# Attention's loads in step order, the first w1 in four quarters, one early split of A11, and idle products at the start

## The reference

```python
for t in range(S):                      # decaying linear attention
    state = gamma * state + outer(k[t], v[t])
    y[t] = scale * q[t] @ state
x = y as (1536, 512)
P = sinkhorn(exp(x @ w_gate - max))     # 8 rounds, 8 experts
x = sum_e P[:, e] * (relu(x @ w1[e]) @ w2[e])       # w1 512x1024, w2 1024x512
p = domain_probs / rows' sums                        # 4 experts
out = sum_e p[:, e] * (relu(x @ w1[e]) @ w2[e])
```

## Time and profile before

| | |
|---|---|
| median of 3 runs | 1560.71 us (1558.86 to 1561.56) |
| the profiled execution: its time | 1563.57 us |
| its span | 1561.8 us |
| PE busy | 1548.5 us, 99% of the span |
| DVE, ACT, POOL busy | 56%, 29%, 3% |
| attention (to the first product of the experts) | 55.5 us |

### The profile page before, as it was taken

How to read it: one execution, slowest core, us unless ns; L and a number is a source line. 1 busy time by engine, 2 the same in 40 slices (tenths; PEclk the granted TensorE clock), 3 DMA queues, 4 the chain that set the end, 5 groups by cost and what they waited for, 6 DMA issues and landing times.

```text
span 1561.8 us, 21255 instructions
## 1 busy us (share of the span) xinstructions
PE 1548.5 (99%) x8228; PEld 1405.0 (90%) x8228; DVE 881.9 (56%) x1434; ACT 445.8 (29%) x860; POOL 53.3 (3%) x45
## 2 busy tenths in 40 slices
PE   8999999999999999999999999999999999999999
PEld 7888998899889988998999899988998899889988
DVE  5846756546545555464555554667555546455553
ACT  4421322223213222232133122333322223213321
POOL 4400000000000000000000000012000000000000
PEclk9999999999999999999999999999999999999999
DMA  9201001011010010010110100101001011011011
GB/s 318 98 0 55 27 28 55 3 52 55 1 54 30 23 54 26 27 54 0 54 54 0 54 27 28 55 0 55 29 26 55 19 36 54 0 54 54 1 43 66
DMA packets 34699, 67.28 MB, mean 43 GB/s; under 512 B 2256, under 2 KB 2384, under 8 KB 34640
## 3 DMA queue, kind: packets, MB, share of 16 engines
q1 hardware_dynamic: 34064, 66.16, 12.2%
q10 hardware_dynamic: 576, 0.30, 0.1%
HBM read 63.31 MB, written 3.15 MB: 43 GB/s over the span
## 4 chain that ended last, share of the span: by engine, by line
PE 97%; DMA 1%; DVE 1%; ACT 0%; SPq 0%; issue 0%; POOL 0%; DVEq 0%; POOLq 0%
PE bank L1066 17%; PE bank L1065 17%; PE bank L1064 17%; PE bank L1043 15%; PE bank L1047 15%; PE bank L1045 15%; DMA qt_in<-in_q_t 1%; PE bank L926 1%; PE bank L964 1%; DMA k_in<-in_k 0%; PE bank L946 0%; PE bank L1011 0%; PE bank L958 0%; DVE w_lo L625 0%; PE bank L992 0%; PE bank L994 0%
## 5 line engine op out<-in xcount | busy, mean ns | idle before, releaser
L1043 PE MATMUL bank<-x_hi,w_hi 128*128 128x384 f32 x1344 | 450.5, 335 | 4.2 <-DVE w_lo L625 2.3
L1047 PE MATMUL bank<-x_hi,w_lo 128*128 128x384 f32 x1344 | 450.2, 335 | 0.0
L1045 PE MATMUL bank<-x_lo,w_hi 128*128 128x384 f32 x1344 | 450.0, 335 | 0.0
L1066 PE MATMUL bank<-w_hi,h_lo 128*128 128x512 f32 x1152 | 449.2, 390 | 0.0
L1065 PE MATMUL bank<-w_lo,h_hi 128*128 128x512 f32 x1152 | 449.0, 390 | 0.0
L1064 PE MATMUL bank<-w_hi,h_hi 128*128 128x512 f32 x1152 | 448.5, 389 | 0.0
L789 DVE SCALAR_TENSOR_TENSOR acc<-bank,gate,acc 128x512 f32<-128x512 f32 x252 | 189.2, 751 | 374.7 <-PE bank L1066 374.7
L490 ACT COPY ups<-bank 128x384 f32<-128x384 f32 x288 | 138.0, 480 | 908.3 <-PE bank L1047 908.3
L742 DVE TENSOR_TENSOR ups<-bank,ups 128x384 f32<-128x384 f32 x288 | 155.3, 554 | 189.5 <-ACT ups L490 167.8
L1043 PEld LDWEIGHTS bank<-x_hi,w_hi 128*128 128x128 f32 x1344 | 252.9, 188 | 6.9 <-issue 2.6
L1066 PEld LDWEIGHTS bank<-w_hi,h_lo 128*128 128x128 f32 x1152 | 216.2, 188 | 45.0
(11 more groups left out here) (83 smaller groups left out, 503.0 us busy)
## 6 DMA issues: line engine op xcount, KB each, us to landing
w_raw<-in_moe_w SPq DMA_DIRECT2D x47, 1024.0 KB, 5.1
kt_in<-in_k_t SPq DMA_DIRECT2D x12, 256.0 KB, 3.7
qt_in<-in_q_t SPq DMA_DIRECT2D x12, 256.0 KB, 5.8
v_in<-in_v SPq DMA_DIRECT2D x12, 256.0 KB, 6.2
k_in<-in_k SPq DMA_DIRECT2D x10, 256.0 KB, 6.7
out<-acc SPq DMA_DIRECT2D x2, 768.0 KB, 3.5
out<-acc SPq DMA_DIRECT2D x6, 256.0 KB, 2.0
w_first<-in_moe_w SPq DMA_DIRECT2D x1, 1024.0 KB, 5.1
```

The source lines that it names most:

```text
L1043: nc.tensor.matmul(o, w1_hi[:, w, kc, fs], x_hi[:, x, kc, at], start=start and kc == 0, stop=False, skip_group_check=True)
L1045: nc.tensor.matmul(o, w1_hi[:, w, kc, fs], x_lo[:, x, kc, at], start=False, stop=False, skip_group_check=True)
L1047: last = nc.tensor.matmul(o, w1_lo[:, w, kc, fs], x_hi[:, x, kc, at], start=False, stop=kc == 1, skip_group_check=True)
L1066: last = nc.tensor.matmul(o, h_lo[:, f, b, rows], w2_hi[:, f, :], start=False, stop=(n == UC - 1))
```

## The change

1. SP loads in step order: kt, qt, k, v of step s together. `rise` moves from ACT's queue to SP's, ahead of step 2's loads.
2. The first w1 comes as four quarters of 256 KB (128 rows each, semaphore `w1_first`), one behind the loads of each of steps 5 to 8.
3. `warm(n)`: three idle products (`WARM_GAP`) behind score(0), three behind score(1).
4. POOL: `first_w1_sum(0)` ahead of raise_q(10), (1) and (2) behind it, (3) behind raise_q(11). The memset of wg_parts is first in its program.
5. A11 is split by itself: ACT `first_w1_high(0)` behind step 9's state copy (ahead of x_high1(4)), DVE `first_w1_low(0)` behind mask_scores(11), and `up` waits for `a11_ready` for its first product, S2, S3 and S1 get shares of their own.
6. The gate weights' split (ACT and DVE) goes to the beginning, gate2's row sums to behind the third half.

```diff
-WARM = 8
+WARM, WARM_GAP = 8, 3
...
             load_qk(0, 0)
+            load_k(0, 0)
             sp.dma_start(mask[:, :, :, :], ...).then_inc(mask_in, 16)
+            load_v(0, 0)
             for s in range(1, STEPS):
                 c, b = s // BATCH, s % BATCH
-                if s == 8:
-                    load_w1(moe_w1, 0, 0)
+                if s == 2:
+                    sp.dma_start(rise[1][:, :, :], ...).then_inc(rise_in, 16)
                 if c > 1:
                     sp.wait_ge(y_done, s - 4 + 1)
                 load_qk(c, b)
-                load_kv((s - 1) // BATCH, (s - 1) % BATCH)
-            load_kv(CH - 1, 1)
+                load_kv(c, b)
+                if 5 <= s < 5 + DC:
+                    at = slice((s - 5) * P, (s - 4) * P)
+                    sp.dma_start(w1_raw[:, s - 5, :], moe_w1[0, at, 0:UF]).then_inc(w1_first, 16)
...
+            for s in range(BATCH, STEPS - BATCH):
+                raise_q(s)
+                decay_k(s)
+            first_w1_sum(0)
+            raise_q(STEPS - 2)
+            first_w1_sum(1)
+            first_w1_sum(2)
+            raise_q(STEPS - 1)
+            first_w1_sum(3)
             sums_low(CH - 1)
...
+            def first_w1_high(part):
+                if part == 0:
+                    act.wait_ge(w1_first, 16 * DC)
+                    nc.scalar.copy(w1_hi[:, W_A11, :, :], w1_raw[:, 0:2, 0:2 * P]).then_inc(a11_hi, 1)
...
+                if s == STEPS - 3:
+                    first_w1_high(0)
...
+                if s == STEPS - 2:
+                    first_w1_low(0)
+                if s == STEPS - 1:
+                    first_w1_low(1)
+                    first_w1_low(2)
...
-            split_w1_low(0, 0)
-            split_w1_low(0, 1)
             x_low0(CH - 1)
...
             score(0)
+            warm(WARM_GAP)
             for s in range(STEPS):
                 if s < STEPS - 1:
                     score(s + 1)
+                if s == 0:
+                    warm(WARM_GAP)
                 attend(s)
...
-                    if p == 0:
+                    if p == 0 and not first:
                         pe.wait_ge(w1_ready, ...)
+                    elif first and n == 0:
+                        pe.wait_ge(a11_ready, 1)
+                    elif first:
+                        pe.wait_ge(w1_ready, {W_S2: 1, W_S3: 1, W_S1: 2, W_S4: 3}.get(w, 4))
```

More of the change, by code:

```diff
@@ L179, in retention_moe_moe_kernel @@
         pool_chain = sem("pool_chain")
+        w1_first = sem("w1_first")
+        a11_hi = sem("a11_hi")
+        a11_ready = sem("a11_ready")
         w1_in = sem("w1_in")
@@ L349, in sums_low, with first_w1_sum @@
                                         ALU.subtract).then_inc(x_lot, 1)
+            def first_w1_sum(n):
+                a11, a21 = w1_raw[:, 0:2, 0:2 * P], w1_raw[:, 0:2, 2 * P:4 * P]
+                a12, a22 = w1_raw[:, 2:4, 0:2 * P], w1_raw[:, 2:4, 2 * P:4 * P]
+                s2, s3, s4 = w1_sum[:, 0, :, :], w1_sum[:, 1, :, :], w1_sum[:, 2, :, :]
+                if n == 0:
+                    pool.wait_ge(w1_first, 16 * DC)
+                else:
+                    pool.wait_ge(w1_summed, n)
+                if n == 0:
+                    nc.gpsimd.tensor_tensor(s3, a11, a21, ALU.subtract).then_inc(w1_summed, 1)
+                elif n == 1:
+                    nc.gpsimd.tensor_tensor(a21, a21, a22, ALU.add).then_inc(w1_summed, 1)
+                elif n == 2:
+                    nc.gpsimd.tensor_tensor(s2, a21, a11, ALU.subtract).then_inc(w1_summed, 1)
+                else:
+                    nc.gpsimd.tensor_tensor(s4, a12, s2, ALU.subtract).then_inc(w1_summed, 1)
+            nc.gpsimd.memset(wg_parts[:, :, :].bitcast(F32), 0.0).then_inc(wg_zeroed, 1)
             pool.wait_ge(kdecay_in, 16)
@@ L452, in split_w1_high, with gate_weights @@
                                    col_halves[:, 2:4, :, :]).then_inc(w1_hi_ready, 1)
+            def gate_weights():
+                act.wait_ge(wg_in, 16)
+                act.wait_ge(wg_zeroed, 1)
+                nc.scalar.copy(wg_parts[:, :, 0:E1], wg_raw[:, :, :]).then_inc(wg_hi_ready, 1)
             act.wait_ge(zeroed, 1)
             nc.scalar.copy(act_warm[:, 1:2], act_warm[:, 0:1])
+            gate_weights()
             for s in range(STEPS):
@@ L458, in _ @@
                 if s == STEPS - 1:
-                    split_w1_high(0, 0, first=True)
+                    first_w1_high(1)
+                    first_w1_high(2)
                 if b == 1:
@@ L493, in hidden_high @@
                 nc.scalar.activation(h_hi[:, f, b, :], src, ACT.Relu).then_inc(h_hi_ready, 1)
[L495 to L498, removed]
             def unit(k, p, x2=None, first=False):
@@ L640, in w1_sums, with first_w1_low @@
                 nc.vector.tensor_tensor(s4, a12, s2, ALU.subtract).then_inc(w1_summed, 1)
+            def first_w1_low(part):
+                if part == 0:
+                    dve.wait_ge(a11_hi, 1)
+                    low(w1_lo[:, W_A11, :, :], w1_raw[:, 0:2, 0:2 * P], w1_hi[:, W_A11, :, :]).then_inc(a11_ready, 1)
+                elif part == 1:
+                    dve.wait_ge(w1_hi_ready, 1)
+                    low(w1_lo[:, W_S2:W_S3 + 1, :, :], w1_sum[:, 0:2, :, :],
+                        w1_hi[:, W_S2:W_S3 + 1, :, :]).then_inc(w1_ready, 1)
+                else:
+                    dve.wait_ge(w1_hi_ready, 2)
+                    low(w1_lo[:, W_S1, :, :], w1_raw[:, 0:2, 2 * P:4 * P], w1_hi[:, W_S1, :, :]).then_inc(w1_ready, 1)
             def split_w1_low(k, part):
@@ L678, in _ @@
             mask_scores(0)
+            dve.wait_ge(wg_hi_ready, 1)
+            low(wg_parts[:, :, E1:2 * E1], wg_raw[:, :, :], wg_parts[:, :, 0:E1]).then_inc(wg_lo_ready, 1)
             for s in range(STEPS):
@@ L698, in _, with gate2_rows @@
             split_w1_low(0, 3)
[L699 to L707, removed]
+            def gate2_rows():
+                dve.wait_ge(gate2_in, 16)
+                then_wait(nc.vector.reduce_sum(row_sum[:, :], gate2[:, :, :], axis=AX.X))
+                then_wait(nc.vector.tensor_scalar_add(row_sum[:, :], row_sum[:, :], EPS))
+                then_wait(nc.vector.reciprocal(row_sum[:, :], row_sum[:, :]))
+                then_wait(nc.vector.tensor_tensor(gate2[:, :, :], gate2[:, :, :],
+                                                  row_sum[:, :].unsqueeze(2).to_broadcast([P, NSUB, E2]), ALU.mult))
             def gate_logits():
@@ L967, in attend, with warm @@
                 last.then_inc(y_done, 1)
+            def warm(n):
+                for i in range(n):
+                    nc.tensor.matmul(bank[7][:, 0:P], state[1][:, 0, :], state[1][:, 0, :], start=True, stop=True)
             pe.wait_ge(zeroed, 4)
-            for i in range(WARM):
-                nc.tensor.matmul(bank[7][:, 0:P], state[0][:, 0, :], state[0][:, 0, :], start=True, stop=True)
+            warm(WARM)
             score(0)
+            warm(WARM_GAP)
             for s in range(STEPS):
```

37 lines of the change are left out of this document (12 added, 25 removed).

## The result

The changed kernel took 1556.5 us in the median of 9 runs (1555.95 to 1557.1) against 1560.7 us (1558.86 to 1562.22, 9 runs) for the kernel before: a ratio of 0.9974 with a 95% interval of 0.9964 to 0.9984, 4.2 us less. The forecast was 1554.5 in a range of 1552.6 to 1558.6, so the time lies in the range, faster as forecast, by two thirds of the 6.2 us. On two later occasions, with new runs of both, the difference was 3.1 and 3.3 us (ratio 0.9980, interval 0.9970 to 0.9989, 10 runs of the change; ratio 0.9982, interval 0.9973 to 0.9991, 11 runs).

What follows compares the result with a forecast made beforehand. PE, busy 99% of the span, bounds the kernel: its work, idle stretches and low clock. Terms 0.9 + 1.6 - 0.3 + 2.3 + 1.7 + 0 = 6.2 us, off the median 1560.7, gave 1554.5 us, range 1552.6 to 1558.6.

Steps and rivals of the forecast that it cites:

- A22's product: End of the first up: PE's wait for DVE, 1.0 us before, about stays; 0 us counted.
- From the median, 1560.7 - 6.2: Last step: the 6.2 us summed from the profiled execution's ledger, taken off the median, giving 1554.5 us.
- start of attention: First scores: idle products and a later qt cost, filled gaps and a full clock give back; 0.9 us gained.
- waits for loads in mid-attention: At score(8): with w1 in quarters qt lands in time and PE's wait goes; 1.6 us gained.
- end of attention: ACT's A11 copy and POOL's third sum delay the last mask, so attention ends 0.3 us later.
- wait for w1's low part: Before the first up: A11's low part is ready before attention's last product, so PE's wait goes; 2.3 us gained.
- clock behind it: Behind attention, 55 to 60 us: without the idle 2.3 us PE's clock doesn't fall; 1.7 us gained.
- rival B: Steps 5 to 9 stay bound by loads at 278 GB/s, 3.7 us of waiting: 1558.2 us; chance 0.15.
- Now A11 needs no sum ... The wait goes: +2.3: End of attention: A11, split without a sum, is ready before attention's last product; 2.3 us gained.
- A: Rival: PE's clock falls at the start, 10 to 15 us, all the same: 1556.7 us; chance 0.17.
- C: Rival: POOL's low part doesn't disturb DVE, first up's end wait goes, 1.0 us more: 1553.5 us; chance 0.13.
- D: Rival: all attention bound by loads, below a mean 296 GB/s; slower, 1565.1 us; chance 0.05.

Runs made afterwards that it cites:

- r_before: The kernel before, unchanged, profiled for a second trace: one execution, 1559.9 us, span 1558.1 us.
- e_w1whole_2: The changed kernel with the first w1 as one 1,024 KB DMA ahead of step 8's loads: 1557.62 us, beside the changed kernel's 1556.87.
- e_a11joined: The changed kernel with A11 and S1 split together again by ACT and DVE: 1557.06 us, against 1556.9 for the changed kernel beside it.
- e_lowdve: The changed kernel with the low part of the last chunk's sums on DVE, not POOL: 1556.21 us, 0.7 below the changed kernel beside it.
- e_nogap: The changed kernel without the six idle products behind score(0) and score(1): 1557.35 us (1556.21 to 1559.21).
- e_before_filled: The kernel before with idle products alone: three behind score(0), three behind score(1), eight after attention: 1559.61 us against 1560.0, ratio 0.9994.
- r_after: The changed kernel, unchanged, run again for a second trace: 1556.9 us (1556.68 to 1557.87).

## Why the prediction was right, and where its size was off

**The steps against the first trace were right.** Forecast first, measured in brackets: score(1) at 9.8 (9.72), the third score at once (so), no wait at score(8) with qt at 6.5 us (none, 5.5), attention into the first up at 51.0 (50.92), no fall of the clock in either place (none), A22's product at 64.5 (64.12). The span of the trace was to be 1561.8 - 6.2 = 1555.6 and is 1555.2. Of the parts, the wait before score(1) was 1.63 and not 0.7, made up for by a shorter score(0).

**The step that failed is the last one: "From the median, 1560.7 - 6.2".** I took what the profiled execution could give back from a median 2.9 us below that execution. It was that much longer for a reason, and the reason was in the terms. r_before shows it. In the right column stand differences of measured times, in the middle one the forecast, with what was seen where it differs:

| term | against the first trace | against r_before |
|---|---|---|
| start of attention | +0.9 | -1.5 (scores without a wait, clock full; the products and the load order cost) |
| waits for loads in mid-attention | +1.6 (+1.4 seen) | +0.2 (0.4 in step 7, less the change's 0.2) |
| end of attention | -0.3 (-0.15 seen) | -0.15 |
| wait for w1's low part | +2.3 | +2.3 |
| clock behind it | +1.7 (+1.6 seen) | +1.6 |
| A22's product | 0 (+0.4 seen) | +0.4 |
| sum | 6.2 forecast, 6.6 seen | 2.9 = 1558.1 - 1555.2 |

The right column's first entry: attend(0) began at 10.18 in r_before and at 11.68 in the change. The last four rows can be checked in two pieces: from step 9's update of the state (k_dec·v) to the first up took 9.2 us in both traces of the kernel before and 7.0 in the change, and from the first up to the end 1506.3 in both and 1504.3 in the change. The rows are rounded; measured stretch by stretch the sums are 6.6 and 2.9. So the terms at the end of attention are the same in both, and the terms of loads and starting clock lie between -1.3 and +2.3 by execution. The median's 3.1 to 4.2 us lies between the columns.

What was mis-sized most is the clock. The forecast took two falls, 3.4 us, out of a median whose run has one: 31 of 81 runs of the kernel before lost less than half a fall, and only 15 lost about two or more. Between runs that kept their clock, the change gains 2.0 us (1558.9 against 1556.9), which is about the wait for w1's low part; the clock adds 1.1 to 1.3 in the median. "1.6 us gained" at score(8) measured 0.75 in the median (e_w1whole_2), and "Sum: ... 0.9 us gained" at the start was right for one execution and wrong in sign for another. That the time lies in the range, with a sum 2.0 to 3.1 us too large, is in part luck: the upper end, 1558.6, was set for rival B's loads and not for this.

**A wrong credit:** "Now A11 needs no sum ... The wait goes: +2.3" was right in size and mostly wrong in cause. e_a11joined gives 1.8 of it to POOL's sums moved forward (1.1, which the prediction named as not being work) and DVE's order (0.7), and shows that what A11's own split gains ends in the wait before A22's product.

**The rivals.** A and B did not come in any of the change's three traces, and A in none of its 30 runs. C came by hand: e_lowdve took away that wait for 0.7 us, forecast 1.0. D was far off at 352 to 390 GB/s; the rate at which it decides, by its own terms, is 294 and not 296. The Trainium skill's rule for DMAs of 1 MiB and more (page "DMA: Bandwidth & Descriptors", section "Bandwidth"), by which four quarters should be slower than one load, is not borne out by this kernel: whole, w1 is 0.75 us slower. The fixed 2.0 us that the prediction put beside the rule stand in that page's section "Anatomy of one DMA — SWDGE (gpsimd) path", for DMAs issued from GpSimd, and the rule's measurements are of such DMAs too; the loads here are issued from SP.

## What to carry to other kernels

Before subtracting gains worked out of one trace from a median, compare that trace's own time with the median: if it is 2.9 us above, then waits for DMAs and stretches at low clock in it are suspects, and each of them needs a second trace. A wait between engines that is in both traces, here the 2.3 us for w1's low part, is the safer term. A fall of the clock is not, even in two traces of two: look at the granted clock of every run on record, which here showed 31 of 81 runs without a full one.

An early phase that is bound by its loads gave nothing here for another order of them or for fewer instructions beside them, but it holds free room on PE: products that only keep the clock up are nearly free there (e_nogap), while they cost 0.7 us where PE had no gap to fill (e_before_filled). They buy an even time more than a low one.

Time gained on PE counts only up to the next place where PE waits for another engine: A11's own split gained 0.4 us at the first up and lost it again 13 us later.

When an operation of DVE on SBUF is nearly three times too long, look at POOL first. Moving a small piece of elementwise work off POOL can be faster even when DVE is the busier engine.

## What the runs showed of the hardware that I had not expected

- **POOL and DVE.** With POOL's 128x1024 subtraction at 57.05 to 60.09, two casts of DVE, which have one SBUF input, took 3.50 us instead of 1.29, and POOL's operation 3.04 where it had taken 2.40. The split of 32 elements, which took 2.38 us beside POOL in the earlier trace rows, takes 0.18 at 8.86 us in the change, where POOL is idle. I had expected it only of DVE operations with two SBUF inputs, as I wrote. The Trainium skill, page "GPSIMD Engine Reference", section "Specifications", names both kinds (two SBUF inputs, or a mode that uses both ports); the trace agrees.
- **The clock at the start** is not the same in two executions of one program: the kernel before ran 10 to 15 us at 0.66 in one and at 1.00 in the other. Its gaps differed too (0.8 and 0.8 us, and 0.7 alone), so this doesn't show that equal gaps can give both. Eight idle products took between 3.41 and 3.79 us in all the traces, and score(0) behind them 1.16 us in two traces of the change and 2.08 in the third, all at a PEclk of 1.00; what makes score(0) longer is not shown.
- **One load landed late.** k and v of step 3 in the change, issued at 9.07 and 9.54 us, the last number being the time to landing:

```profile
k_in<-in_k SPq DMA_DIRECT2D x1, 256.0 KB, 7.4
...
v_in<-in_v SPq DMA_DIRECT2D x1, 256.0 KB, 8.8
```

They landed 1.9 us apart, where k and v of the two steps before are 0.7 apart, and where the same two are 0.7 apart in r_after. A 16 KB load of the instruction queue (q8) ran in between 15.8 and 17.1 us:

```profile
q8 instruction: 1, 0.02, 5.4%
```

A share of 5.4% of 16 engines over 1.3 us is 1.1 us of one engine, about the delay. That such loads cause the varying waits is argued from this one place and wasn't tried; r_before has such late loads at other places, k of two other steps landed 1.9 and 2.4 us behind the load ahead of it instead of 0.7.
